# Pooled attention and channel mix on one core: the first queries are loaded ahead of the first keys, and the start's order of work is changed

## What is computed

```python
q_pool = q.reshape(B, H, S // 2, 2, D).mean(axis=3)     # B 4, H 8, S 1152, D 64
scores = scale * np.matmul(q_pool, k.transpose(0, 1, 3, 2))
scores = scores - np.max(scores, axis=-1, keepdims=True)
attn = np.exp(scores)
attn = attn / (np.sum(attn, axis=-1, keepdims=True) + 1e-09)
out = np.matmul(attn, v)                                 # 576 queries for each head
# heads side by side: x is [4, 576, 512]
xn = (x - mu) / np.sqrt(var + 1e-06) * g_ln
x + np.maximum(xn @ w_ch1, 0.0) @ w_ch2                  # w_ch1 512 x 2048, w_ch2 2048 x 512
```

## Time and profile before

| | |
|---|---|
| median of 3 runs | 834.38 us (834.36 to 834.64) |
| profiled execution | 834.26 us |
| its span (first to last instruction) | 832.4 us |
| busy, share of the span | PE 98%, PEld 83%, DVE 55%, ACT 40%, POOL 43% |
| DMA traffic | 58.52 MB, mean 70 GB/s |
| chain of work that ended last, by engine | PE 90%, DVE 6%, ACT 2%, issue 1%, DMA 1% |

### The profile page before, as it was taken

The page is one execution under the profiler, slowest core; times in us unless marked ns, Lnnn a source line. Parts: engine busy times, 40 slices in busy tenths (PEclk is TensorE's granted clock), DMA queues, the critical chain, the costliest instruction groups (busy, mean ns, idle before and its releaser), DMA issues.

```text
span 832.4 us, 16182 instructions
## 1 busy us (share of the span) xinstructions
PE 818.8 (98%) x6676; PEld 692.7 (83%) x6676; DVE 461.5 (55%) x705; ACT 332.6 (40%) x715; POOL 359.2 (43%) x252
## 2 busy tenths in 40 slices
PE   8999999999999999999999999999999999999998
PEld 6877777877777777778779999999999999999997
DVE  5788898889998888988354542222123223122112
ACT  3665566765665765566634421211121121111110
POOL 2788999998898888888730000000000000000000
PEclk9999999999999999999999999999999999999999
DMA  5865445564444655301213410000001001001001
GB/s 128 183 168 131 94 106 122 141 142 118 91 107 111 142 142 138 89 2 30 81 51 127 127 39 1 1 13 26 1 1 39 1 1 39 1 1 38 1 1 39
DMA packets 30808, 58.52 MB, mean 70 GB/s; under 512 B 8208, under 2 KB 18704, under 8 KB 27152
## 3 DMA queue, kind: packets, MB, share of 16 engines
q1 hardware_dynamic: 29520, 56.90, 27.2%
q10 hardware_dynamic: 1216, 0.59, 0.3%
HBM read 52.76 MB, written 4.72 MB: 69 GB/s over the span
## 4 chain that ended last, share of the span: by engine, by line
PE 90%; DVE 6%; ACT 2%; issue 1%; DMA 1%; SPq 0%; ACTq 0%; DVEq 0%
PE banks L983 24%; PE banks L996 23%; PE banks L554 17%; PE banks L543 11%; PE banks L487 4%; PE banks L541 3%; DVE pm L810 2%; DVE acc_end L834 2%; PE banks L570 2%; PE banks L612 1%; ACT pT L718 1%; PE banks L495 1%; PE banks L581 1%; PE banks L249 1%; DMA k_in_rows<-in_k_dram 1%
## 5 line engine op out<-in xcount | busy, mean ns | idle before, releaser
L429 POOL TENSOR_TENSOR acc<-acc,pT 128x576 f32<-128x576 f32 x160 | 237.7, 1486 | 23.0
L983 PE MATMUL banks<-xT,weights 128*128 128x384 f32 x1152 | 216.7, 338 | 0.3 <-DVE weights L1045 0.3
L996 PE MATMUL banks<-weights,hT 128*128 128x512 f32 x864 | 210.7, 389 | 0.0
L983 PEld LDWEIGHTS banks<-xT,weights 128*128 128x128 f32 x1152 | 201.6, 188 | 7.0 <-DVE weights L1045 0.8
L1054 DVE SCALAR_TENSOR_TENSOR hT<-banks,hT 128x384 fp32r<-128x384 f32 x96 | 53.5, 557 | 274.4 <-ACT hT L1033 274.4
L718 ACT ACTIVATE pT<-banks 128x576 f32<-128x576 f32 x288 | 171.9, 653 | 37.8 <-PE banks L541 32.7
L996 PEld LDWEIGHTS banks<-weights,hT 128*128 128x128 f32 x864 | 160.9, 188 | 26.9
L810 DVE TENSOR_REDUCE pm<-banks 128x2 f32<-128x1024 f32 x128 | 153.7, 1221 | 42.1 <-PE banks L487 40.8
L1033 ACT ACTIVATE hT<-banks 128x384 fp32r<-128x384 f32 x96 | 47.2, 492 | 323.6 <-PE banks L983 323.6
L543 PE MATMUL banks<-qT,kT 64*128 64x288 f32 x1728 | 162.3, 298 | 4.3 <-DVE pm L810 3.5
L543 PEld LDWEIGHTS banks<-qT,kT 64*128 64x128 f32 x1728 | 133.5, 184 | 19.3 <-DVE pm L810 8.7
(11 more groups left out here) (85 smaller groups left out, 528.7 us busy)
## 6 DMA issues: line engine op xcount, KB each, us to landing
q_in_rows<-in_q_dram SPq DMA_DIRECT2D x56, 284.0 KB, 6.6
k_in_rows<-in_k_dram SPq DMA_DIRECT2D x56, 284.0 KB, 5.3
vn<-in_v_dram SPq DMA_DIRECT2D x16, 576.0 KB, 5.1
wstage<-in_moe_w_ch_dram SPq DMA_DIRECT2D x32, 256.0 KB, 2.8
out_dram<-x SPq DMA_DIRECT2D x16, 256.0 KB, 2.1
k_in_rows<-in_k_dram SPq DMA_DIRECT2D x4, 288.0 KB, 4.7
q_in_rows<-in_q_dram ACTq DMA_DIRECT2D x2, 256.0 KB, 4.9
q_in_rows<-in_q_dram SPq DMA_DIRECT2D x2, 256.0 KB, 4.0
```

The source lines that it names most:

```text
L429: nc.gpsimd.tensor_tensor(total, pT[:, h % 2, 0] if kt == 1 else total, pT[:, h % 2, kt], ALU.add).then_inc(chained, 1)
L983: last = nc.tensor.matmul(ps_h[f % 2][:, 0:CW], weights[:, 2 * f, a, c * 128:(c + 1) * 128], xT[:, par, b, c], start=m == 0, stop=m == len ...
L996: last = nc.tensor.matmul(ps_y[kk], hT[:, f % 2, a, kk * 128:(kk + 1) * 128], weights[:, 2 * f + 1, b], start=f == 0 and m == 0, stop=f == ...
```

## The change

Loads: SP issues first the 512-query parts of pair 0 (`query_tiles`), then the first four tiles (512 keys) of both heads' keys, which count on a new semaphore `k_first`. ScalarE's queue has the queries' rests and the other five tiles of keys (`k_in`), with no wait ahead. Then ScalarE makes a copy of one column, in front of which its table is loaded. SP sends pair 1's queries ahead of pair 1's keys.

Order: pair 0's `KQ` comes ahead of `KA`. `KA` signals after its first four tiles; the ninth key tile is transposed behind the queries' copy. ScalarE copies the queries, then the first 512 key columns, then the other 512, the last 128, the rest queries, and then makes the plain copies, the queries' first. The first `M` waits for the queries' copy and the first 512 key columns, the second for the next 512, the ninth for the last 128. In `FIRST_STEPS` 12 `W` are left of 26. In pair 0 alone (`PAIR_0`) two `M` of pair 1 come before the first `S`, and the banks of some `S` change.

```diff
-    FIRST_STEPS = ("KA@0 W@7 KQ@2 W@7 W@7 W@7 M@4 M@6 W@2 W@2 M@4 W@2 W@2 M@6 W@2 W@2 M@4 KA@0 W@2 M@6 W@2 W@2 M@4 "
-                   "W@2 W@2 M@6 KQ@0 W@2 M@4 W@2 W@2 L@6 E@2 W@0 W@0 W@0 W@0 W@0 W@0 SH@3 W@0 W@0")
+    FIRST_STEPS = ("KQ@2 W@7 W@7 KA@0 W@7 M@4 M@6 M@4 W@2 M@6 W@2 M@4 KA@0 M@6 W@2 M@4 W@2 M@6 KQ@0 M@4 W@2 L@6 E@2 "
+                   "W@0 W@0 W@0 W@0 SH@3")
+    PAIR_0 = PAIR_STEPS.replace("M@4 S@6 S@2 S@0 M@4 S@6 S@2 M@0", "M@4 M@0 S@6 S@2 S@4 S@6 S@2 M@0", 1)
...
+        def query_tiles(eng, j, s):
+            eng.dma_start(qn[:, 0:FULL, s].rearrange("p t r d -> p t (r d)"),
+                          q_v[j // BP, 2 * (j % BP) + s]).then_inc(q_in, 16)
+
+        def query_rest(eng, j, s):
+            eng.dma_start(qn[0:REST, FULL, s].rearrange("p r d -> p (r d)"),
+                          q_m[j // BP, 2 * (j % BP) + s]).then_inc(q_in, 16)
+
+        def first_keys(eng, part, loaded):
...
+            first, last = (0, GW // 128) if part == 0 else (GW // 128, KT)
+            for s in range(2):
+                eng.dma_start(kn[:, first:last, s], k_v[0, s, :, first:last]).then_inc(loaded, 16)
...
-            load_keys(0)
+            for s in range(2):
+                query_tiles(sp, 0, s)
+            first_keys(sp, 0, k_first)
+            sp.wait_ge(q_summed, 1)
+            load_queries(sp, 1)
             load_keys(1)
-            for j in range(1, 3):
-                sp.wait_ge(q_summed, j)
-                load_queries(sp, j)
+            sp.wait_ge(q_summed, 2)
+            load_queries(sp, 2)
...
         def turn_first_keys(pe, j):
-            pe.wait_ge(k_in, 32 * (j + 1))
+            pe.wait_ge(*((k_first, 32) if j == 0 else (k_in, 32 * (j + 1))))
             for kt in range(KT - 1):
+                if j == 0 and kt == GW // 128:
+                    last.then_inc(first_turned, 1)
+                    pe.wait_ge(k_in, 32)
                 last = nc.tensor.transpose(flat(pair_banks("KA", j))[:, kt * 128:(kt + 1) * 128],
                                            kn[:, kt].rearrange("p s d -> p (s d)"), ident[:])
             last.then_inc(ka_turned, 1)
+            if j == 0:
+                pe.wait_ge(q_hi, 1)
+                turn_last_keys(j)
...
-            if at == 0:
+            if n == 0:
+                pe.wait_ge(q_hi, 1)
+                pe.wait_ge(first_hi, 1)
+            elif n == 1:
+                pe.wait_ge(ka_hi, 1)
+            elif n == MAXES - 1:
+                pe.wait_ge(kb_hi, 1)
+            elif at == 0:
...
+            def first_keys_hi():
+                dst, src = kT[:, 0, 0], flat(pair_banks("KA", 0))
+                act.wait_ge(first_turned, 2)
+                nc.scalar.copy(dst[:, 0:GW], src[:, 0:GW]).then_inc(first_hi, 1)
+                act.wait_ge(ka_turned, 1)
+                nc.scalar.copy(dst[:, GW:(KT - 1) * 128], src[:, GW:(KT - 1) * 128]).then_inc(ka_hi, 1)
+                last_keys_hi(0)
+                queries_rest(0)
+                copy_first_queries(0)
+                copy_first_keys(0)
+
+            def first_queries_hi():
+                act.wait_ge(first_turned, 1)
+                nc.scalar.copy(qT[:, 0, 0], flat(pair_banks("KQ", 0))[:, 0:NQ]).then_inc(q_hi, 1)
...
-            act.wait_ge(zeros_made, 1)
-            load_queries(act, 0)
+            for s in range(2):
+                query_rest(act, 0, s)
+            first_keys(act, 1, k_in)
+            act.wait_ge(ident_made, 2)
+            nc.scalar.copy(zs[:, 0:1], one[:])
             act.wait_ge(zeros_made, 2)
             act.wait_ge(ones_made, 3)
```

More of the change, by code:

```diff
@@ L100, in pair_steps @@
         seen = {}
-        for kind, bank in parsed(PAIR_STEPS if j + 1 < PAIRS else PAIR_END):
+        for kind, bank in parsed(PAIR_0 if j == 0 else PAIR_STEPS if j + 1 < PAIRS else PAIR_END):
             at = seen.get(kind, 0)
@@ L197, in pooled_attention_channel_mix @@
                                                         sem("ones_made"))
-        q_in, k_in, v_in = sem("q_in"), sem("k_in"), sem("v_in")
+        q_in, k_in, v_in, k_first = sem("q_in"), sem("k_in"), sem("v_in"), sem("k_first")
+        first_turned, first_hi = sem("first_turned"), sem("first_hi")
         w_in = [sem(f"w_in{r}") for r in range(RING)]
@@ L296, in load_queries @@
                     continue
[L297 to L300, removed]
+                query_tiles(eng, j, s)
+                query_rest(eng, j, s)
         def keys_loaded(j):
@@ L461, in turn_first_keys, with turn_last_keys @@
             last.then_inc(ka_turned, 1)
+            if j == 0:
+                pe.wait_ge(q_hi, 1)
+                turn_last_keys(j)
+        def turn_last_keys(j):
+            nc.tensor.transpose(flat(pair_banks("KQ", j))[:, QW:QW + 128],
+                                kn[:, KT - 1].rearrange("p s d -> p (s d)"), ident[:]).then_inc(kq_turned, 1)
         def turn_queries(pe, j):
-            pe.wait_ge(k_in, 32 * (j + 1))
             pe.wait_ge(q_summed, j + 1)
@@ L467, in turn_queries @@
             for t in range(QT):
-                nc.tensor.transpose(dst[:, t * 128:(t + 1) * 128], qs[:, t].rearrange("p s d -> p (s d)"), ident[:])
-            nc.tensor.transpose(dst[:, QW:QW + 128], kn[:, KT - 1].rearrange("p s d -> p (s d)"),
-                                ident[:]).then_inc(kq_turned, 1)
+                last = nc.tensor.transpose(dst[:, t * 128:(t + 1) * 128], qs[:, t].rearrange("p s d -> p (s d)"),
+                                           ident[:])
+            if j == 0:
+                last.then_inc(first_turned, 1)
+            else:
+                pe.wait_ge(k_in, 32 * (j + 1))
+                turn_last_keys(j)
         def score_maxima(pe, n):
             j, at = n // MAXES, n % MAXES
-            if at == 0:
+            if n == 0:
[6 more added lines that the diff above has]
+            elif at == 0:
                 pe.wait_ge(ka_hi, j + 1)
@@ L674, in keys_hi, with last_keys_hi, queries_rest @@
                 nc.scalar.copy(kT[:, j % 2, 0, 0:(KT - 1) * 128], flat(pair_banks("KA", j))).then_inc(ka_hi, 1)
+            def first_keys_hi():
[11 more added lines that the diff above has]
+                nc.scalar.copy(qT[:, 0, 0], flat(pair_banks("KQ", 0))[:, 0:NQ]).then_inc(q_hi, 1)
+            def last_keys_hi(j):
+                act.wait_ge(kq_turned, j + 1)
+                nc.scalar.copy(kT[:, j % 2, 0, (KT - 1) * 128:SEQ],
+                               flat(pair_banks("KQ", j))[:, QW:QW + 128]).then_inc(kb_hi, 1)
             def queries_hi(j):
                 act.wait_ge(kq_turned, j + 1)
+                nc.scalar.copy(qT[:, j % 2, 0], flat(pair_banks("KQ", j))[:, 0:NQ]).then_inc(q_hi, 1)
+                last_keys_hi(j)
+                queries_rest(j)
+            def queries_rest(j):
                 src = flat(pair_banks("KQ", j))
-                nc.scalar.copy(qT[:, j % 2, 0], src[:, 0:NQ]).then_inc(q_hi, 1)
-                nc.scalar.copy(kT[:, j % 2, 0, (KT - 1) * 128:SEQ], src[:, QW:QW + 128]).then_inc(kb_hi, 1)
                 rest = slice(FULL * 128, FULL * 128 + REST)
@@ L728, in scalar_step @@
                     exponential(n)
+                elif kind == "KA" and n == 0:
+                    first_keys_hi()
+                elif kind == "KQ" and n == 0:
+                    first_queries_hi()
                 elif kind == "KA":
@@ L734, in scalar_step @@
                     queries_hi(n)
[L735 to L738, removed]
+                    if n == 1:
+                        copy_first_queries(1)
                 elif kind == "SH":
```

## The result

| | before | after |
|---|---|---|
| median | 834.37 us (834.23 to 834.64, 4 runs) | 827.59 us (827.47 to 828.16, 4 runs) |
| profiled execution, its span | 834.26, 832.4 us | 827.5, 825.7 us |

The ratio is 0.992 with a 95% interval of 0.9903 to 0.9937: 6.8 us faster, where 5.4 were forecast. 827.59 lies on the lower end of the forecast's range, 827.6. The mean granted clock is listed as 0.999 or 1.000 in all four runs.

The account below looks back on a forecast made before the run. TensorE, busy 98% of the span, bounds the kernel, leaving the chain of waits from 0 to 30 us. First score 5.2 us earlier plus 0.2 in pair 0 gives 5.4: 834.38 to 829.0 us, range 827.6 to 831.7.

Parts of the forecast that it names:

- Part 1: First loads: queries at the head of SP's queue let the query sum start at 6.8 us instead of 8.20.
- The rival that order gives nothing: First loads: queries land no sooner, both queues sharing the same engines; time 830.4 us; chance 12%.
- Part 2: From query sum to first maximum: first maximum at 11.2 us, 0.9 us earlier.
- The hidden table load: Within part 2: ScalarE loads its table by about 4.8 us, off the path; unhidden it would cost 1.28 us.
- Part 3: Nine maxima, rest and join: 1.15 us per maximum, 12.3 us against 15.97; join ends at 23.5, 4.6 earlier.
- the rival of the round trip: In the maxima: the round trip between two banks keeps them at 1.45 us, not 1.15; 831.7 us; chance 9%.
- Part 4: From join to first scores: `SH` at 23.65 (0.45 gained), first score at 25.2 us, 5.2 us earlier.
- Part 5: Pair 0: a second maximum put ahead leaves the scores, gaining 0.2 us, bounds 0 and 0.5.
- nothing was given back: Rival in pair 0: something not starting earlier bounds it and the gain is given back, 834.2 us; chance 4%.
- The clock: TensorE's clock over the start: removing 14 of 26 transpose steps costs nothing, TensorE working 0.9 of every 1.15 us.
- the two clock rivals: Start: clock falls briefly, 831 to 832 us, 5%; or stays at 1.2 GHz through the maxima, 838.2 us, 4%.

Follow-up runs that it names:

- a_keys_sp: Changed kernel with keys at the head of SP's queue and queries at the head of ScalarE's, no wait ahead; 832.06 us (830.16 to 832.72).
- a_keys_behind: Changed kernel with all keys on SP's queue behind the queries, only the two 32 KB rests on ScalarE's; 828.67 us, single run.
- d_keys_first: Changed kernel with all keys at the head of SP's queue, then the queries' tiles, only the rests on ScalarE's; 831.96 us, single run.
- a_old_w: Changed kernel with the 26 `W` steps of the kernel before at their old places; 831.68 us (831.42 to 832.21).
- B: The kernel before the change; median 834.37 us.
- a_no_pair0: Changed kernel with the old order in pair 0 (one maximum ahead of the first score, not two); 827.70 us (827.54 to 827.87).
- A: The changed kernel; median 827.59 us.
- a_no_w: Changed kernel without any `W` step, the 24 transposes ahead kept; 831.13 us (829.54 to 831.25).
- b_thin: Kernel before with 12 of its 26 `W` steps, at the changed kernel's places in the old order; 831.37 us (830.46 to 833.02).
- b_thin_fill: Kernel before with few `W` steps, some on bank 7 set into the waits behind the first and second maximum; 834.05 us (832.47 to 835.31).
- a_no_table: Changed kernel without ScalarE's early one-column copy, so the table loads ahead of the queries' copy; 828.53 us (828.39 to 829.72).

## Why the prediction was right, and where it was not

The parts in the middle were right. That the number still fell into the range is partly luck: the landing lay outside its own bounds, and a part with the wrong sign took back some of it.

- **Part 1, the loads: the mis-sized term.** Forecast: the sum at 6.8, bounds 5.7 to 8.2. Measured 5.17. I took the pace of the whole load, 176 KB/us, and the keys' place with 64 KB less. But the head of SP's queue had been slowed by the queries beside it and by its smaller packets. With the small rests at the head of the other queue it moved 245 KB/us, and its 512 KB were there at 4.8; the sum then waited for a rest of 32 KB until 5.17. My bound of 4.9 us from issue to landing was of 576 KB in 256-byte packets too, so the 5.7 worked out from it was no bound for queries: 5.17 lies below. `a_keys_sp`, `a_keys_behind` and `d_keys_first` show this. The rival that order gives nothing is refuted.
- **Part 2: right.** 4.47 us against 4.4. The hidden table load: right that it is hidden; uncovered it costs 0.9 at most and not 1.28, since the queries' copy waits for the table while the keys are still being turned.
- **Part 3: right, to 0.03 us.** The reduces are 1.15 apart, and `a_old_w` shows that the transposes had paced them, which refutes the rival of the round trip. The keys of pair 1 made their transposes wait 0.23 us, within the 0 to 0.6 I gave them.
- **Part 4: right within 0.1.** `SH` follows by 0.22 and not 0.15: the 16 transposes wait for bank 0 (the 0.35 in the row at 20.29) and end after the join.
- **Part 5: the sign was wrong.** Pair 0 became 0.27 longer (23.71, 23.44 before), not 0.2 shorter. These 0.47 us took back nearly a third of what the early queries gave beyond the forecast. The first score starts as soon as its shifts are there. The second, on banks 2 and 3, waits for the turned maxima in bank 3 to be read, and ScalarE's last shift ends at 24.31 (23.69 + 0.62). From `SH` to this second score are 2.27 us, and 2.28 in B (28.70 to 30.98), where only the first came later. So 0.26 of part 4 were a milestone's and not the time's. That bank 3 is what holds it is read from the order of steps; the profile names no releaser there. `a_no_pair0` shows that the order does nothing here.
- **Behind it** nothing was given back: pair 1's first score is 6.50 earlier, the end of the span 6.7. Of this, 0.34 arose in pair 1 (24.44 us, 24.78 before), which the prediction did not have and no run explains.
- **The clock: the cost was right, the reason only in part.** A's clock stayed at full speed. The prediction's ground was 0.9 us of work in every 1.15 of the maxima, and the 12 steps left make half of that; `a_no_w` shows that it needs them, for without them the gain is 3.2 us and not 6.8. But there is no `W` between A's first three maxima. That stretch (1.94 of 3.00 us busy) was not looked at, and that it held is luck as far as the prediction goes: the waits of 0.79 and 1.09 us after which B's thin order loses the clock could have been read from the order of the copies. The chances of 5% and 4% for the two clock rivals look low beside the kernels here that lost it in their profiled execution (`a_no_w`, `a_keys_sp`, `b_thin`, `b_thin_fill`, `d_keys_first`). The rule weighed there (the Trainium skill, "TensorE: Matmul & The Clock Gate", "Part 4: PE-mode transpose": transposes do not count as TensorE being busy) does not hold for the transposes of this kernel: A and `a_no_w` differ in them alone, and the mean clock is 0.999 or 1.000 in A's four runs and 0.989 to 0.994 in the five of `a_no_w`.

Taken one at a time out of A, the extra transposes cost 4.1 us (`a_old_w`), the table load 0.9 (`a_no_table`) and the place in the queues 2.6 where the clock held (`a_keys_sp`, its two fastest runs). That is 7.6 and not 6.8: the pieces overlap, pair 0 gives 0.27 back, and how the rest divides was not measured.

## What to carry to other kernels

The time of the start is a chain of few steps, and from the rows of each step its stretches were forecast to 0.1 us here. The landing of a load was missed by 1.6 us, because the row it was taken from had other packets and other traffic beside it. All loads that one wait covers have to be followed: the smallest one landed last. Work that has no use but to hold the clock should be thinned where it makes others wait, not removed, and looked at over several runs, because a clock that falls in some of them shows as a wide spread. Before a step is put on a bank for its freedom, look how wide its neighbours' steps are.

## What was not expected of the hardware

- The clock falls without any long wait: in `a_no_w` TensorE's matmuls had no wait above 0.91 us ahead of the first fall at 13.2 (0.91, 0.64 and 0.63 ahead of the maxima), with 4.13 of 6.80 us busy; in A the longest behind the first transposes is 1.06 us, without a fall.
- Half of the granted clock doubles a transpose's pitch (eight in 1.94 or 1.06 us), but a fall costs less than that suggests: the profile of `a_no_w` has 3.4 and 6.7 us at 1.2 GHz and is only 2.0 us above A, and one of 6.83 us in `b_thin` goes with 2.6 us between its slowest and its fastest run. That VectorE's 1.15 us per maximum cover part of it is my explanation, not a test.
- The moment at which the clock first rises differs between executions: in A's profile the weight loads fall from 230 to 141 ns at about 5.1 us and the 24 transposes end in time for the queries at 6.14; in `a_keys_behind` they still take 231 ns at 6.2 and hold the queries until 6.62. Now that the queries come at 6.0, the warm-up itself has come on the path; fewer than 24 were not tried with the `W` steps kept.
